# A fused filter and two-layer feed-forward kernel: the square moved to ScalarE in the first phase, one place of side work per pair

## The reference, cut to what matters

```python
w = exp(weight - max(weight)); w = w / (sum(w) + 1e-9)      # 8 heads x 7 taps
x = sum over k of w[head, k] * x_padded[:, s + k, :]        # causal filter
h = x @ w_in                                                # layer 1: 192 -> 2048
g = where(h >= 1, h, where(h <= -1, 0, (h + 1) ** 2 / 4))
x = g @ w_out                                               # 2048 -> 192
h = x @ w2_in                                               # layer 2
g = s * relu(h) ** 2 + b
out = g @ w2_out
```

## Time and profile before

| | |
|---|---|
| median of three runs | 1143.05 us |
| the profiled execution's own time | 1137.14 us |
| its span, first to last instruction | 1135.1 us |
| PE busy in the span | 1122.6 us (99%) |
| VectorE (DVE) busy | 864.0 us (76%) |
| ScalarE (ACT) busy | 684.8 us (60%) |
| GpSimd (POOL) busy | 3.4 us |
| mean granted TensorE clock | 0.998 |

### The profile page before, as it was taken

The page is one execution under the profiler, slowest core; times in us unless marked ns, Lnnn a source line. Parts: engine busy times, 40 slices in busy tenths (PEclk is TensorE's granted clock), DMA queues, the critical chain, the costliest instruction groups (busy, mean ns, idle before and its releaser), DMA issues.

```text
span 1135.1 us, 23149 instructions
## 1 busy us (share of the span) xinstructions
PE 1122.6 (99%) x9754; PEld 916.6 (81%) x9754; DVE 864.0 (76%) x780; ACT 684.8 (60%) x678; POOL 3.4 (0%) x16
## 2 busy tenths in 40 slices
PE   8999999999999999999999999999999999999998
PEld 4778888888888888888888888888888888888886
DVE  7998978777787777877678777787777877766655
ACT  5667765566654765557565666546655566665543
POOL 1000000000000000000000000000000000000000
PEclk9999999999999999999999999999999999999999
DMA  5112200000001000000000000001000000000000
GB/s 158 29 39 65 57 1 1 29 29 1 1 1 29 29 1 1 1 29 29 1 1 1 29 29 1 1 2 56 1 1 1 1 29 1 1 1 1 29 1 28
DMA packets 12741, 21.32 MB, mean 19 GB/s; under 512 B 1136, under 2 KB 5488, under 8 KB 12656
## 3 DMA queue, kind: packets, MB, share of 16 engines
q1 hardware_dynamic: 12576, 19.99, 6.0%
q0 software_dynamic: 64, 0.00, 0.0%
q10 hardware_dynamic: 16, 0.00, 0.0%
HBM read 13.70 MB, written 6.29 MB: 18 GB/s over the span
## 4 chain that ended last, share of the span: by engine, by line
PE 95%; DVE 3%; issue 1%; ACT 0%; ACTq 0%; DVEq 0%
PE acc L773 30%; PE h L726 30%; PE acc_rem L788 20%; PE h L739 15%; DVE g_lo L509 1%; PE acc L882 1%; DVE g L488 1%; DVE g L490 0%; PE h L865 0%; DVE mixed_rem L568 0%; ACT r L319 0%; DVE mixed_rem L547 0%; DVE dn_lo L598 0%; DVE up_rem_lo L598 0%; PE h L829 0%
## 5 line engine op out<-in xcount | busy, mean ns | idle before, releaser
L493 DVE SCALAR_TENSOR_TENSOR g<-r,scale,h 128x1024 f32<-128x1024 f32 x128 | 161.8, 1277 | 95.4 <-ACT r L322 95.4
L341 ACT ACTIVATE g_hi<-g,shift 128x1024 fp32r<-128x1024 f32 x128 | 147.6, 1153 | 117.4 <-PE acc_rem L788 108.3
L319 ACT ACTIVATE r<-h,half 128x1024 f32<-128x1024 f32 x128 | 138.0, 1112 | 123.1 <-PE h L739 120.2
L322 ACT ACTIVATE r<-h 128x1024 f32<-128x1024 f32 x128 | 127.4, 1025 | 127.2 <-PE h L739 123.8
L773 PE MATMUL acc<-g_hi,dn_hi 64*128 64x512 f32 x1024 | 200.5, 388 | 0.4 <-issue 0.4
L773 PE MATMUL acc<-g_lo,dn_hi 64*128 64x512 f32 x1024 | 200.2, 388 | 0.0
L788 PE MATMUL acc_rem<-g_hi,dn_rem 64*128 64x512 f32 x1024 | 199.9, 387 | 0.0
L773 PE MATMUL acc<-g_hi,dn_lo 64*128 64x512 f32 x1024 | 199.4, 386 | 0.0
L788 PE MATMUL acc_rem<-g_lo,dn_rem 64*128 64x512 f32 x1024 | 199.3, 386 | 0.0
L726 PE MATMUL h<-x_rem,up_rem_hi 64*128 64x512 f32 x1016 | 198.5, 387 | 0.0
L512 DVE SCALAR_TENSOR_TENSOR g_lo<-g,shift,g_hi 128x1024 fp32r<-128x1024 f32 x128 | 164.0, 1281 | 37.3 <-ACT g_hi L341 37.3
(11 more groups left out here) (114 smaller groups left out, 1344.9 us busy)
## 6 DMA issues: line engine op xcount, KB each, us to landing
xraw<-in_x SPq DMA_DIRECT2D x7, 518.0 KB, 4.3
out<-res SPq DMA_DIRECT2D x7, 512.0 KB, 3.3
stage<-in_moe_w_out SPq DMA_DIRECT2D x5, 384.0 KB, 3.4
xraw_rem<-in_x SPq DMA_DIRECT2D x14, 129.5 KB, 4.0
out<-res_rem SPq DMA_DIRECT2D x7, 256.0 KB, 3.6
stage<-in_moe_w_in SPq DMA_DIRECT2D x6, 256.0 KB, 5.3
stage<-in_moe_w_in SPq DMA_DIRECT2D x2, 512.0 KB, 4.8
y<-in_moe_w_out SPq DMA_DIRECT2D x2, 384.0 KB, 4.5
```

The costliest lines, as they stand in the source:

```text
L319: nc.scalar.activation(r[k][:], h[k][:], ACT.Relu, scale=0.5, bias=half[:, 0:1]).then_inc((r_ready, odd_relu_done)[k], 1)
L322: nc.scalar.activation(r[k][:], h[k][:], ACT.Relu).then_inc(r_ready, 1)
L341: nc.scalar.activation(g_hi[k][:], g[k][:], ACT.Identity, bias=shift[:, 0:1]).then_inc(hi_ready, 1)
L493: nc.vector.scalar_tensor_tensor(g[k][:], r[k][:], scale[:, 0:1], h[k][:], ALU.mult, ALU.mult).then_inc(h_used, 1)
```

## The change

**Phase 0, elementwise.** Chunks 0, 1 and 14 keep the form with two VectorE passes; all the others (2 to 13 and 15) take the square on ScalarE. In the first pair the order on VectorE is maximum 0, maximum 1, second 0, second 1. The later phases keep even and odd as they were.

**Phase 0, side work.** VectorE's side work moves to one place per pair, ahead of the maximum of the even chunk (`early`); the taps 0 of block 1 move to ScalarE (`tap0`), VectorE keeps 12 passes (`mix_second`). Layer 1's weights are cut into 12 pieces instead of 10, and their staging and waits are renumbered.

**Opening.** `warm` is set to 0.5 over 512 columns instead of zero over 256; the warm-up is one matmul of 256 and one of 128 columns instead of three of 256 and one more. The taps are spread unnormalized; the reciprocal of their sum is spread by two matmuls of one column and applied as the scale of the rounding passes. Four instead of two taps of the rest channels stand ahead of the wait for the half that TensorE filters. After the first pair TensorE does 7 steps of two extra matmuls (`keep_busy`), into a PSUM tile that is overwritten later.

```diff
-        W1 = [("up", 0, HEAD), ("up_rem", 0, HEAD), ("up", HEAD, HALF), ("up_rem", HEAD, HALF), DN[0],
-              ("up", HALF, FF), ("up_rem", HALF, FF)] + DN[1:]
+        W1 = [("up", 0, HEAD), ("up_rem", 0, HEAD), ("up", HEAD, 2 * HEAD), ("up_rem", HEAD, 2 * HEAD), DN[0],
+              ("up", 2 * HEAD, HALF), ("up_rem", 2 * HEAD, HALF), ("up", HALF, FF), DN[1], ("up_rem", HALF, FF),
+              DN[2], DN[3]]
+        FIRST_TWO = (0, 1, CH - 2)
+            return j in FIRST_TWO if opening(blk) else j % 2 == 0
...
-            for n in range(6, 10):
-                sp.wait_ge(w1_lo_done, parts(0, n - 3))
+            for n, free in ((8, 5), (9, 4), (10, 7), (11, 8)):
+                sp.wait_ge(w1_lo_done, parts(0, free))
                 load_w(0, n)
-            sp.wait_ge(mix_step, 2 * TAPS)
+            sp.wait_ge(second_mix, 2 * (TAPS - 1))
             load_x(2)
...
+            def tap0(part):
+                if part == 0:
+                    act.wait_ge(x_loaded, 48)
+                    act.wait_ge(taps_scaled, 2)
+                    act.wait_ge(x_rem_lo_done[0], 1)
+                    nc.scalar.activation(mixed_rem[:], xraw_rem[:, 0:T], ACT.Copy,
+                                         scale=taps[:, 1, 0:1]).then_inc(tap0_done, 1)
+                else:
+                    act.wait_ge(x_lo_done[0], 1)
+                    act.wait_ge(w1_lo_done, parts(0, 2))
+                    nc.scalar.activation(mixed[:], xraw[:, :, 0:T], ACT.Copy,
+                                         scale=taps[:, 0, 0:1]).then_inc(tap0_done, 1)
...
                     elif j % 2 == 0:
-                        round_g(layer, S0 + j - 1, 1, None)
-                    relu(layer, S0 + j, j % 2)
-                    if layer == 0 and j % 2:
-                        square_odd(G0 + j // 2 + 1)
+                        round_g(layer, S0 + j - 1, 1, seconds(j - 1))
+                    for f in (early or {}).get(j, ()):
+                        f()
+                    relu(layer, S0 + j, j % 2, two(j))
+                    if not two(j):
+                        square(j % 2, relu_count(blk, j))
...
+            act.wait_ge(sums_spread, 1)
+            nc.scalar.activation(taps[:, :, TAPS:TAPS + 1], spread_sum, ACT.Copy).then_inc(sums_ready, 1)
...
-            weights_hi(0, 2)
+            for n in (2, 3):
+                weights_hi(0, n)
             act.wait_ge(mixed_pe_done, 1)
-            nc.scalar.activation(X2[0][:, 1, :], mixed_pe, ACT.Copy).then_inc(mixed_pe_hi, 1)
-            for n in (3, 4):
+            nc.scalar.activation(X2[0][:, 1, :], mixed_pe, ACT.Copy,
+                                 scale=taps[:, 0, TAPS:TAPS + 1]).then_inc(mixed_pe_hi, 1)
+            for n in (4, 5, 6):
                 weights_hi(0, n)
...
-            weights_hi(0, 5)
+            weights_hi(0, 7)
...
-            for j, n in ((2, 6), (3, 7), (6, 8), (9, 9)):
+            for j, n in ((1, 8), (3, 9), (5, 10), (9, 11)):
                 e[j].append(lambda n=n: weights_hi(0, n))
-            e[8].append(lambda: round_mixed_rem(1, X1, None))
-            e[13].append(lambda: round_mixed(1, X1, None))
-            phase(0, None, 0, 0, 0, extras=e)
+            e[1].append(lambda: tap0(0))
+            e[5].append(lambda: tap0(1))
+            e[9].append(lambda: round_mixed_rem(1, X1, None))
+            phase(0, None, 0, 0, blk=0, early={14: [lambda: round_mixed(1, X1, None)]}, extras=e)
...
                     elif j % 2 == 0:
                         low(layer, S0 + j - 1, 1)
-                    first(layer, S0 + j, j % 2)
+                    for f in (early or {}).get(j, ()):
+                        f()
+                    first(layer, S0 + j, j % 2, two)
+                    if j == 1 and layer == 0 and opening(blk):
+                        second(S0, 0)
+                        second(S0 + 1, 1)
                     if j % 2:
                         low(layer, S0 + j - 1, 0)
...
-            nc.vector.memset(warm[:, 0:2 * P], 0.0).then_inc(warm_set, 1)
+            nc.vector.memset(warm[:], 0.5).then_inc(warm_set, 1)
...
-            for k in range(1, 3):
+            for k in range(1, 5):
                 mix_first_rem(k)
             dve.wait_ge(mixed_pe_hi, 1)
-            nc.vector.tensor_tensor(X2[1][:, 1, :], mixed_pe, X2[0][:, 1, :].bitcast(F32),
-                                    ALU.subtract).then_inc(mixed_pe_lo, 1)
-            for k in range(3, TAPS):
+            nc.vector.scalar_tensor_tensor(X2[1][:, 1, :], mixed_pe, taps[:, 0, TAPS:TAPS + 1],
+                                           X2[0][:, 1, :].bitcast(F32), ALU.mult, ALU.subtract).then_inc(mixed_pe_lo, 1)
+            for k in range(5, TAPS):
                 mix_first_rem(k)
             weights_lo(0, 1)
-            low_mixed_rem(0, X2)
-            for n in (2, 3):
...
+            for part in range(2):
+                nc.vector.tensor_scalar(taps[:, part, 0:TAPS], taps[:, part, 0:TAPS], taps[:, part, TAPS:TAPS + 1], None,
+                                        ALU.mult).then_inc(taps_scaled, 1)
+            for n in (2, 3, 4):
                 weights_lo(0, n)
...
-            e = mixing(1, lambda part, k: 6 + max(1, k) if part else (2, 3, 3, 4, 5, 5, 6)[k])
-            e.setdefault(1, [])
-            for j, n in ((1, 4), (2, 5), (3, 6), (4, 7), (7, 8), (10, 9)):
-                e[j].append(lambda n=n: weights_lo(0, n))
-            e[9].append(lambda: low_mixed_rem(1, X1))
-            e[14] = [lambda: low_mixed(1, X1)]
-            phase(0, None, 0, 0, extras=e)
+            w = lambda n: lambda: weights_lo(0, n)
+            m = lambda part, k: lambda: mix_second(part, k)
+            e = {2: [w(5), w(6)],
+                 4: [w(7), w(8), m(0, 1)],
+                 6: [w(9), m(0, 2), m(0, 3), m(0, 4)],
+                 8: [m(0, 5), m(0, 6), m(1, 1), m(1, 2)],
+                 10: [lambda: low_mixed_rem(1, X1), w(10), m(1, 3)],
+                 12: [m(1, 4), m(1, 5), m(1, 6)],
+                 14: [w(11), lambda: low_mixed(1, X1)]}
+            phase(0, None, 0, 0, blk=0, early=e)
...
+            def keep_busy(xs, steps):
+                for _ in range(steps):
+                    for t, rows in enumerate(HALVES):
+                        nc.tensor.matmul(acc_rem[:, t, :], up_hi[0][rows, 0:P], xs[0][rows, t, :],
+                                         start=True, stop=True)
...
                         first_pair(xs)
+                        keep_busy(xs, 7)
...
-            warm_up(3)
-            pe.wait_ge(taps_step, 6)
+            warm_up(2 * P)
+            warm_up(P)
+            pe.wait_ge(taps_exp, 1)
             pe.wait_ge(head_of_step, 5)
...
-            warm_up(1)
-            pe.wait_ge(taps_step, 7)
+            pe.wait_ge(taps_step, 5)
+            for part in range(2):
+                last = nc.tensor.matmul(spread_sum[:, part, :], head_of[:, part * P:(part + 1) * P],
+                                        head_taps[:, TAPS:TAPS + 1], start=True, stop=True)
+            last.then_inc(sums_spread, 1)
+            pe.wait_ge(taps_step, 6)
...
-            w_up = {2: parts(0, 4), 2 * QCH: parts(0, 7)}
-            w_dn = {0: parts(0, 5), QCH: parts(0, 8), 2 * QCH: parts(0, 9), 3 * QCH: parts(0, 10)}
+            w_up = {2: parts(0, 4), QCH: parts(0, 7), 2 * QCH: parts(0, 10)}
+            w_dn = {0: parts(0, 5), QCH: parts(0, 9), 2 * QCH: parts(0, 11), 3 * QCH: parts(0, 12)}
```

More of the change, by code:

```diff
@@ L144, in build @@
         r_ready = sem("r_ready")
-        odd_relu_done = sem("odd_relu_done")
+        relu_done = [sem(f"relu_done{n}") for n in range(2)]
         h_used = sem("h_used")
@@ L244, in _ @@
             load_x_first()
-            for n in range(6):
+            for n in range(8):
                 load_w(0, n)
@@ L311, in _, with relu @@
         def _(act):
-            def relu(layer, S, k):
+            def relu(layer, S, k, two=True):
                 act.wait_ge(h_ready, S + 1)
@@ L388, in weights_hi, with phase, two, seconds @@
                     nc.scalar.activation(hi, cols, ACT.Copy).then_inc((w1_hi_done, w2_hi_done)[layer], 1)
-            def phase(layer, before, S0, P0, G0=None, blk_before=None, extras=None, last=None):
+            def phase(layer, before, S0, P0, blk=None, blk_before=None, early=None, extras=None):
+                def two(j):
+                    return layer == 1 or two_pass(blk, j)
+                def seconds(j):
+                    return g_count(blk, j) if layer == 0 and two(j) else None
                 for j in range(CH):
@@ L480, in _, with first @@
         def _(dve):
-            def first(layer, S, k):
+            def first(layer, S, k, two=True):
                 dve.wait_ge(r_ready, S + 1)
@@ L486, in first @@
                     dve.wait_ge(lo_ready, S - 1)
-                if layer == 0 and k == 0:
+                if layer == 0 and two:
                     nc.vector.tensor_tensor(g[k][:], h[k][:], r[k][:], ALU.max).then_inc(h_used, 1)
@@ L608, in phase @@
```

(20 more changed lines are left out.)

124 lines of the change are left out of this document (80 added, 44 removed).

## The result

Over 14 runs each the changed kernel takes 1139.51 us (1139.42 to 1140.19) and the kernel before 1142.07 us (1140.59 to 1143.18). The ratio is 0.998, with a 95% interval of 0.9973 to 0.9987: 2.56 us faster by the medians. The profiled executions seem to say the opposite: 1139.49 us (span 1137.4) after, 1137.14 (span 1135.1) before.

What follows compares the result with a forecast made beforehand. VectorE bounds phase 0 in places, a dependent chain the opening, TensorE the rest. Relu 14's 2.85 us gain less 0.1 for piece 8 gives 2.7: 1143.05 to 1140.35 us; range 1139.5 to 1141.3, 8 in 10 1138.4 to 1142.9.

Steps and rivals of the forecast that it cites:

- The opening: Everything before relu of chunk 0: copy of the taps 1.0 us earlier, relu 0 at 18.8 instead of 20.77, gaining 1.95 us.
- The scale in the rounding passes: Opening's rounding passes, now applying the reciprocal of the taps' sum as scale: claimed to cost nothing visible.
- The rate of TensorE: Tap filter's 14 matmuls: switch from slow to fast level after about 4 us; filter ends at 13.3 or 13.8 us.
- The clock after the first pair: TensorE at 20 to 28 us: extra steps leave 0.65 us idle, so the clock holds instead of falling to 0.50.
- Piece 8: ScalarE's weight split in the first pair: load takes 4.4 us, wait 0.1 us, bounds nothing and 2.1 us.
- the slower case: Kernel measured slower than before: chance 0.06, from a late weight load in the first pair and anything overlooked.
- The wait at down(8): Phase 0, chunk 8: TensorE newly waits 2.1 us for VectorE's split of the third down quarter, bounds 0.9 and 2.3.
- Rivals 2 to 4: No wait at down(8), chance 0.12; ScalarE stuck at piece 8's split, 0.08; opening gaining 1.0 instead of 1.95 us, 0.15.
- Rival 1: Clock falls to 0.50 at the new wait before down(8), leaving 1.0 us gained, 1142.0 us; chance 0.25.
- rival 4: Opening gives only 1.0 us instead of 1.95, total gain 1.7 us, 1141.3 us; chance 0.15.
- Relu 14: ScalarE's relu of chunk 14, in phase 0's pair 7: claimed at 80.85 us instead of 83.69, 2.85 us gained.
- The median: Whole kernel: median of the runs falls by 2.7 us, from 1143.05 to 1140.35 us.

Runs made afterwards that it cites:

- b_again: The kernel before, unchanged, timed and profiled a second time; median 1141.88 us, ratio 0.9998, profiled execution 1140.54 us.
- spread_side: w10_early with ScalarE's tap 0 of the large tile moved from after chunk 5 to after chunk 7; median 1135.38 us, ratio 0.9955 to the kernel before.
- no_keep_busy: The changed kernel without the seven extra TensorE steps after the first pair; median 1139.91 us, ratio 0.9984 to the kernel before.
- w10_early: The changed kernel with VectorE's split of the third down quarter before chunk 8 instead of 10, one filter pass swapped; median 1137.62 us, ratio 0.9961 to kernel before.
- odd_squares: The changed kernel with phase 0's elementwise work as before (ScalarE squares for odd chunks only); median 1145.83 us, ratio 1.0033 to the kernel before.
- sq_only: The kernel before with only the squares of chunks 2, 4, 6, 8, 10 and 12 moved to ScalarE; median 1139.0 us, ratio 0.9984.

## Why the prediction was right, point by point

- *The opening* was read correctly. Copy of the taps at 4.16 (4.15 to 4.2 foretold), relu 0 at 18.48 (18.8). The tap filter on TensorE started at 4.92 instead of 5.15, as the two spreads overlap: the second starts at 3.98, in the first one's 1.02 us. The scale in the rounding passes, put at nothing, cost 0.06 to 0.09 us a pass (ScalarE 0.69 and 0.72 us where it took 0.60 and 0.63, VectorE 0.75 where it took 0.69).
- *The rate of TensorE* in the tap filter rose about 4.3 us after the filter's start, as it had done before: it moved with the kernel in this pair of traces. Over all traces it is a matter of chance (6.25 us for the 14 matmuls in b_again, 8.27, 8.40, and 9.10 in spread_side). The Trainium skill, "TensorE: Matmul & The Clock Gate", Part 1, says that the number of slow matmuls varies from run to run; these traces agree.
- *The clock after the first pair* held, and the extra steps are why (no_keep_busy). What was too large is what I thought a fall costs: 1.7 us by the length of the slow stretch, 0.4 to 0.5 measured here, as waits that would have come anyway took up the rest. At down(8), where I had priced it, no fall came, so its price there is not shown.
- *Piece 8*, the ground of the slower case, cost nothing: the load was issued at 19.73 and took 3.7 us (4.4 was foretold), and ScalarE went from chunk 0 to its split at 24.19 with no idle time. Bounded by 0 and 2.1 us, taken as 0.1.
- *The wait at down(8)* came in the pair, on the line and from the split that were named, at 1.65 us instead of 2.1, and w10_early shows that it cost its length. Counted from relu 8 (52.40), ScalarE rounded chunk 9 and VectorE ended the split 0.15 us sooner than the sum had, and TensorE came 0.2 later.
- *Rivals 2 to 4* did not happen: the wait arose, ScalarE had its piece in time, and between these two traces the opening gave more than foretold, 2.3 us. Against b_again it gave 0.2 (18.70 - 18.48), less than rival 4 has: the trace before had the bad case of the opening, which the prediction couldn't know. *Rival 1*, the clock falling at that wait, did not happen either. It did not fall in odd_squares either, after 2.0 us at the same place, while it fell after 1.9 and 2.0 us at the first pair. So the length of the pause alone does not decide; the prediction's counterargument, a weaker stretch ahead of the first pair, agrees with this but was not tested by itself.
- *Relu 14* came at 80.34, 80.85 was foretold: 3.35 us gained in these two traces where the sum had 2.85.
- *The median* moved by 2.56 us, 2.7 was foretold, and that it came so near is partly luck, since two errors met. From the trace that I worked from the gain was 3.35 us, more than the sum had. But that trace was of the bad case of the opening: against b_again relu 14 gained 81.50 - 80.34 = 1.2 us only. The median lies between the two because the runs of the kernel before are a mixture. The changed kernel's opening varies less (relu 0 at 18.48 to 19.16 in the six traces with the new opening, at 18.70 to 20.90 in the four with the old one; its runs lie within 0.8 us, those of the kernel before within 2.6).
- *The failed reading* is the sentence that the profiled execution stands 5.9 us below the median and that I take the difference over. That distance was the rarer, shorter pair of 8.63 us; the changed kernel's profile has no such distance (1139.49 against a median of 1139.51).

## What to carry to other kernels

Before a small gain is summed up from one trace, profile the unchanged kernel twice: here the same program differed by 5.5 us over the steady part and by 2.1 us in the opening. When side work is gathered at one place, check for each piece which engine needs it in the same round; the wait for one 1 us split took back 1.7 of the 2.7 us (relu 0 to relu 14: 62.80 in b_again, 61.86, and 60.1 in w10_early with pairs of equal length) that phase 0 could have given by then. Relieve the full engine first (sq_only, 1.5 us): gathering the work without the relief cost 3.4 us against the kernel before (odd_squares).

## What the runs showed of the hardware

A pair of chunks takes 8.63 or 8.68 us on a TensorE that never stands still. In most traces all pairs of a layer 1 or 2 phase are of one kind; in sq_only and spread_side both kinds alternate within one execution (8.66 us on average in both). One pair of either kind, in the timeline: the first up step, the first down step, and the first up step of the next pair. First the kernel before in its first trace:

```profile
606.71 0.39 PE L726 MATMUL h<-x_hi,up_hi 64*128 64x512 f32 x2
610.79 0.39 PE L773 MATMUL acc<-g_hi,dn_hi 64*128 64x512 f32 x2
615.35 0.39 PE L726 MATMUL h<-x_hi,up_hi 64*128 64x512 f32 x2
```

and in b_again:

```profile
607.35 0.41 PE L726 MATMUL h<-x_hi,up_hi 64*128 64x512 f32 x2
611.43 0.41 PE L773 MATMUL acc<-g_hi,dn_hi 64*128 64x512 f32 x2
616.04 0.40 PE L726 MATMUL h<-x_hi,up_hi 64*128 64x512 f32 x2
```

The 18 up steps take 4.08 us in both, and the 20 down steps, which wait for TensorE's own semaphores between their parts, 4.56 and 4.61. The up steps and the first down steps are 0.227 us apart. In the pair of the first trace the distances after the 11th to the 14th down step are 0.228 to 0.236 us and all others 0.227 or less; in the pair of b_again they are 0.228 to 0.236 from the fifth on. The granted clock is 1.00 in both. What decides between them was not tried and stays open. Over an execution it is worth more than the whole change.
